# A fused convolution and two-layer block: TensorE's products of a step in another order, first-layer and second-layer products alternating

## The reference, cut to what matters

```python
# x (4, 4096, 192); weight_gen (4, 4096, 8 heads, 7 taps); w_in (192, 2048); w_out (2048, 192)
w = exp(weight_gen - max(weight_gen, -1)); w = w / (sum(w, -1) + 1e-9)
out[b, s, h, :] = sum over k of w[b, s, h, k] * x_pad[b, s + k, h, :]     # causal, 24 columns a head
x = out.reshape(16384, 192)
h = x @ w_in                                                             # first layer, 192 -> 2048
g = where(h >= 1, h, where(h <= -1, 0, (h + 1)**2 / 4))                  # gate
return g @ w_out                                                         # second layer, 2048 -> 192
```

## Time and profile before

| | |
|---|---|
| median of three runs | 1261.16 us |
| profiled execution, first to last instruction | 1259.3 us (its own time is not given apart from this span) |
| TensorE products | 1209.8 us, 96% of the span |
| TensorE weight loads | 1094.7 us, 87% |
| VectorE | 818.9 us, 65% |
| ScalarE | 898.3 us, 71% |
| GpSimd | 697.0 us, 55% |
| mean granted TensorE clock | 0.998 |

### The profile page before, as it was taken

How to read it: one execution, slowest core, us unless ns; L and a number is a source line. 1 busy time by engine, 2 the same in 40 slices (tenths; PEclk the granted TensorE clock), 3 DMA queues, 4 the chain that set the end, 5 groups by cost and what they waited for, 6 DMA issues and landing times.

```text
span 1259.3 us, 21159 instructions
## 1 busy us (share of the span) xinstructions
PE 1209.8 (96%) x6932; PEld 1094.7 (87%) x6932; DVE 818.9 (65%) x1434; ACT 898.3 (71%) x1773; POOL 697.0 (55%) x450
## 2 busy tenths in 40 slices
PE   0699999999999999999999999999999999999998
PEld 0578999999999999999999999999999999999987
DVE  1886666666666666666666666666666666666565
ACT  0567777777777777777777777777777777777776
POOL 2496555775555775555776555676555676555500
PEclk9999999999999999999999999999999999999999
DMA  3311111001111101111101111101111100110000
GB/s 116 105 36 48 49 48 48 27 20 47 47 47 47 44 3 47 47 47 47 47 0 47 47 47 47 47 8 39 47 47 47 47 20 27 47 47 12 13 13 13
DMA packets 17426, 51.59 MB, mean 41 GB/s; under 512 B 1800, under 2 KB 8068, under 8 KB 17408
## 3 DMA queue, kind: packets, MB, share of 16 engines
q1 hardware_dynamic: 17264, 51.25, 11.9%
q10 hardware_dynamic: 144, 0.11, 0.0%
HBM read 38.77 MB, written 12.58 MB: 41 GB/s over the span
## 4 chain that ended last, share of the span: by engine, by line
PE 93%; SPq 3%; DVE 3%; DMA 1%; ACT 1%; issue 0%; DVEq 0%
PE slot L581 46%; PE acc L601 44%; PE slot L566 2%; SPq L240 1%; SPq L255 1%; DMA out_raw<-in_moe_w_out 1%; SPq L252 1%; DVE slot L472 1%; DVE gate_low L478 1%; DVE out_parts L515 0%; DVE in_main_low L508 0%; SPq L258 0%; DVE in_rest_low L508 0%; ACT gate_high L375 0%; SPq L223 0%
## 5 line engine op out<-in xcount | busy, mean ns | idle before, releaser
L601 PE MATMUL acc<-out_parts,gate_high 128*128 128x384 f32 x2048 | 616.4, 357 | 6.0 <-DVE gate_low L478 5.9
L478 DVE TENSOR_TENSOR gate_low<-slot,gate_high 128x512 fp32r<-128x512 f32 x512 | 353.7, 691 | 398.9 <-ACT gate_high L375 398.6
L601 PE MATMUL acc<-out_parts,gate_low 128*128 128x192 f32 x2048 | 513.7, 251 | 0.5 <-DVE gate_low L478 0.5
L364 ACT ACTIVATE half_relu<-slot 128x512 f32<-128x512 f32 x512 | 307.7, 601 | 288.5 <-PE slot L581 288.4
L601 PEld LDWEIGHTS acc<-out_parts,gate_high 128*128 128x128 f32 x2048 | 384.9, 188 | 27.1 <-DVE gate_low L478 8.4
L601 PEld LDWEIGHTS acc<-out_parts,gate_low 128*128 128x128 f32 x2048 | 390.3, 191 | 17.9 <-DVE gate_low L478 0.7
L472 DVE SCALAR_TENSOR_TENSOR slot<-slot,square 128x512 f32<-128x512 f32 x512 | 353.0, 690 | 3.9 <-ACT square L370 3.9
L370 ACT ACTIVATE square<-half_relu 128x512 f32<-128x512 f32 x512 | 325.2, 635 | 0.0
L375 ACT ACTIVATE gate_high<-slot 128x512 fp32r<-128x512 f32 x512 | 304.0, 594 | 25.6 <-DVE slot L472 25.4
L301 POOL TENSOR_TENSOR conv<-x_in,tap_w 128x768 f32<-128x768 f32 x31 | 47.8, 1542 | 482.3 <-DVE tap_w L462 468.4
L301 POOL TENSOR_TENSOR tap<-x_in,tap_w 128x768 f32<-128x768 f32 x186 | 289.6, 1564 | 0.0
(11 more groups left out here) (41 smaller groups left out, 493.4 us busy)
## 6 DMA issues: line engine op xcount, KB each, us to landing
x_in<-in_x SPq DMA_DIRECT2D x30, 960.0 KB
out<-out_sb SPq DMA_DIRECT2D x32, 384.0 KB, 2.6
gen_in<-in_weight_gen SPq DMA_DIRECT2D x31, 112.0 KB, 2.3
out_raw<-in_moe_w_out SPq DMA_DIRECT2D x4, 384.0 KB, 9.9
in_main<-in_moe_w_in SPq DMA_DIRECT2D x4, 256.0 KB, 4.7
in_rest<-in_moe_w_in SPq DMA_DIRECT2D x8, 128.0 KB, 7.6
x_in<-in_x SPq DMA_DIRECT2D x1, 768.0 KB
x_in<-in_x SPq DMA_DIRECT2D x4, 139.5 KB
```

The costliest lines, as they stand in the source:

```text
L364: nc.scalar.activation(half_relu[n % 2][:], tile_slot(pair, b, n)[:], ACT.Relu, scale=0.5, bias=0.5).then_inc(relu_done, 1)
L478: nc.vector.tensor_tensor(gate_low[n % 4][:], tile_slot(pair, b, n)[:], gate_high[n % 4][:].bitcast(F32), ALU.subtract).then_inc(gate_low_ ...
L601: ins = nc.tensor.matmul(dst, stationary, moving, start=(n == 0 and j == 0), stop=(n == NT - 1 and j == 1))
```

## The change

The same products with the same operands are issued, as many as before. Only their order on TensorE is another:

- The five first-layer products of tile n and the eight second-layer products of tile n - 3 are now one mixed sequence, `hidden_and_outputs`. Neighbours write different banks, since the blocks of the second layer are staggered too.
- The transposes of `turn` stand behind the whole step. Before, they stood between the step's first and second layer.
- In the two places where only one layer is there (the first three steps of the kernel, the last three tiles) the products stand alone.

```diff
-            def hidden(pair, b, n):
-                slot_free(pe, pair, b, ("tile", n))
...
-                for j, (w, xt) in enumerate(products):
...
-                ins.then_inc(hidden_done, 1)
+            def hidden(pair, b, n, j):
+                if j == 0:
+                    slot_free(pe, pair, b, ("tile", n))
...
+                if j == 4:
+                    ins.then_inc(hidden_done, 1)
+
+            def out_ready(pair, b, n):
                 wait(pe, gate_low_done, pair, 2 * NT, NT * b + n + 1)
...
+            def acc_free(pair, b, n, i):
+                if n == 0:
+                    wait(pe, out_summed, pair, 2 * TOK, TOK * (b - 1) + i + 1)
+
+            def out_both(pair, b, n, i):
+                acc_free(pair, b, n, i)
+                ins = nc.tensor.matmul(acc[i][:, 0:2 * D], gate_high[n % 4][:, i * P:(i + 1) * P],
+                                       out_parts[:, n, :, :].rearrange("p a d -> p (a d)"),
+                                       start=(n == 0), stop=(n == NT - 1))
+                if n == NT - 1:
+                    ins.then_inc(acc_done, 1)
+
+            def out_low(pair, b, n, i):
+                nc.tensor.matmul(acc[i][:, 0:D], gate_low[n % 4][:, i * P:(i + 1) * P],
+                                 out_parts[:, n, 0, :], start=False, stop=False)
...
+            def hidden_and_outputs(pair, b, n, done):
+
+                if done[2] == NT - 1:
+                    hidden(pair, b, n, 0)
+                    out_ready(*done)
+                    out_low(*done, 0)
...
+                    hidden(pair, b, n, 4)
+                    out_low(*done, 2)
+                    out_low(*done, 3)
+                    out_both(*done, 2)
+                    out_both(*done, 3)
+                else:
+                    hidden(pair, b, n, 0)
+                    out_ready(*done)
+                    out_both(*done, 0)
+                    hidden(pair, b, n, 1)
+                    out_low(*done, 0)
+                    hidden(pair, b, n, 2)
+                    out_both(*done, 1)
+                    hidden(pair, b, n, 3)
+                    out_low(*done, 1)
+                    hidden(pair, b, n, 4)
+                    out_both(*done, 2)
+                    out_both(*done, 3)
+                    out_low(*done, 2)
+                    out_low(*done, 3)
...
                     for n in range(NT):
-                        hidden(pair, b, n)
+                        if n >= LAG:
+                            hidden_and_outputs(pair, b, n, (pair, b, n - LAG))
+                        elif not (b == 0 and is_first(pair)):
+                            hidden_and_outputs(pair, b, n, (*before(pair, b), NT + n - LAG))
+                        else:
+                            only_hidden(pair, b, n)
                         if n in turn_after(pair, b):
                             turn(*after(pair, b), turn_after(pair, b).index(n))
-                        if n >= LAG:
-                            outputs(pair, b, n - LAG)
-                        elif not (b == 0 and is_first(pair)):
-                            outputs(*before(pair, b), NT + n - LAG)
```

More of the change, by code:

```diff
@@ L568, in turn @@
                 ins.then_inc(turned, 1)
[L570 to L585 removed]
+            def hidden(pair, b, n, j):
+                if j == 0:
+                    slot_free(pe, pair, b, ("tile", n))
+                    if n == 0:
+                        wait(pe, turned_low_done, pair, 4, 2 * b + 2)
+                    if b == 0 and is_first(pair) and n % CT == 0:
+                        pe.wait_ge(in_low_done, 2 * (n // CT) + 2)
+                w, xt = ((in_main_high, xt_high), (in_main_low, xt_high), (in_main_high, xt_low),
+                         (in_rest_high, xt_rest), (in_rest_low, xt_rest))[j]
+                ins = nc.tensor.matmul(tile_slot(pair, b, n)[:], w[:, n * P:(n + 1) * P], xt[b][:],
+                                       start=(j == 0), stop=(j == 4))
+                if j == 4:
+                    ins.then_inc(hidden_done, 1)
+            def out_ready(pair, b, n):
                 wait(pe, gate_low_done, pair, 2 * NT, NT * b + n + 1)
@@ L590, in outputs @@
                     pe.wait_ge(out_low_done, n // CT + 1)
-                for i in range(TOK):
-                    tokens = slice(i * P, (i + 1) * P)
-                    if n == 0:
-                        wait(pe, out_summed, pair, 2 * TOK, TOK * (b - 1) + i + 1)
-                    low = (acc[i][:, 0:D], gate_low[n % 4][:, tokens], out_parts[:, n, 0, :])
-                    both = (acc[i][:, 0:2 * D], gate_high[n % 4][:, tokens],
-                            out_parts[:, n, :, :].rearrange("p a d -> p (a d)"))
-                    order = (both, low) if n < NT - 1 else (low, both)
-                    for j, (dst, stationary, moving) in enumerate(order):
-                        ins = nc.tensor.matmul(dst, stationary, moving, start=(n == 0 and j == 0),
-                                               stop=(n == NT - 1 and j == 1))
-                    if n == NT - 1:
-                        ins.then_inc(acc_done, 1)
+            def acc_free(pair, b, n, i):
+                if n == 0:
+                    wait(pe, out_summed, pair, 2 * TOK, TOK * (b - 1) + i + 1)
@@ new lines, in outputs @@
+            def outputs(pair, b, n):
+                out_ready(pair, b, n)
+                if n < NT - 1:
+                    out_both(pair, b, n, 0)
+                    out_both(pair, b, n, 1)
+                    out_low(pair, b, n, 0)
+                    out_both(pair, b, n, 2)
+                    out_low(pair, b, n, 1)
+                    out_both(pair, b, n, 3)
+                    out_low(pair, b, n, 2)
+                    out_low(pair, b, n, 3)
+                else:
+                    out_low(pair, b, n, 0)
+                    out_low(pair, b, n, 1)
+                    out_both(pair, b, n, 0)
+                    out_low(pair, b, n, 2)
+                    out_both(pair, b, n, 1)
+                    out_low(pair, b, n, 3)
+                    out_both(pair, b, n, 2)
+                    out_both(pair, b, n, 3)
@@ new lines, in only_hidden @@
+            def only_hidden(pair, b, n):
+                for j in range(5):
+                    hidden(pair, b, n, j)
+            def hidden_and_outputs(pair, b, n, done):
[17 more added lines that the diff above has]
+                    out_ready(*done)
+                    out_both(*done, 0)
+                    hidden(pair, b, n, 1)
+                    out_low(*done, 0)
+                    hidden(pair, b, n, 2)
+                    out_both(*done, 1)
+                    hidden(pair, b, n, 3)
+                    out_low(*done, 1)
+                    hidden(pair, b, n, 4)
[3 more added lines that the diff above has]
+                    out_low(*done, 3)
```

10 lines of the change are left out of this document (removed).

## The result

The changed kernel takes 1325.8 us (median of four runs, 1325.5 to 1327.1) against 1261.0 us before: a ratio of 1.0516, 95% interval 1.0501 to 1.0531. It is slower, as forecast, but 18 us more than the 1308 of the forecast and 2 us outside its range.

What follows compares the result with a forecast made beforehand. The prediction took TensorE, 93% of the span, as the bound, with no waits in the loop. From 1261.2 us it took -4 for pace, +49 for the stall and +2 for the start: 1308.2 us, range 1289 to 1324.

Steps and rivals of the forecast that it cites:

- The stall at a group's start: Steps 2 and 3 of groups 1 to 31: TensorE waits for VectorE's sums, 1.58 us each, +49 us.
- The pace: Ordinary mixed steps: 8 ns gained in each of 509 steps, -4 us, bounds -18 and +8.
- the change of bank is no cheaper than staying: First steps of the kernel: products changing bank cost 0.23 us like the others, so alternation gains near nothing.
- The lower bound: Best case for the pace in ordinary steps: 0.036 us a step gained, -18 us.
- The start: Group 0, waits for `gate_low`: four products now stand behind the wait, +2 us, bounds +0.9 and +4.
- Ordinary tiles: Loop tiles away from group starts: 1.08 us to spare remains, no wait, priced at nothing.
- The clock: TensorE's clock through the new 1.5 us stalls: stays at 1.00 from 110 us on, no cost.
- The first (products become cheaper): Rival, all steps: alternating banks saves 0.15 us a step, -76 us instead of -4, giving 1236 us; chance 0.08.
- The stalls did not lower the clock: Rival, group starts: stalls halve the clock for 3.2 us, 31 times, +50 us, giving 1358 us; chance 0.05.
- the wait does not recur in every step: Rival, ordinary steps: another 0.3 us wait in half of a group's steps, +77 us, giving 1385 us; chance 0.03.
- the stall is there: Rival, group starts: no stall because the sums come earlier than derived, 1257 to 1262 us; chance 0.02.

Runs made afterwards that it cites:

- B0 alone: Kernel before, with only step 3 of every group in the mixed order and the transposes behind it: 1294.7 us.
- H5 alone: Changed kernel with step 3 of every group back in the order of before, the last first-layer product of step 2 staying late: 1285.5 us.
- the transposes alone: Kernel before, with only the transposes moved behind the second layer: 1263.7 us, ratio 1.0019.
- with steps 2 and 3 as before: Changed kernel with steps 2 and 3 of every group in the order of before, layers apart: 1275.0 us.
- the kernel with two blocks: Kernel before, layers apart, with each step's four 384-column products issued first and then its four 192-column products: 1265.2 us.
- batching two tiles: Kernel before, changed to issue two tiles at a time, with eight gate buffers and the sums one step later: 1258.0 us, ratio 0.9972.
- the widened kernels: 192-column products widened to 384 columns: 1400.4 us in the order of before, 1409.2 us in the mixed order (steps 2 and 3 of a group unmixed).
- the mixed kernel with equal lengths: Changed kernel with products 512 columns long (group 0 and tile 15 keep 384) and steps 2 and 3 of a group unmixed: 1580.1 us.

## Why the prediction was wrong

- **The stall at a group's start: right.** +49 forecast; 31 x 1.57 = 48.7 measured by step 3, 50 by the pair of steps. Place, releaser and the number of waits came out, each link of the chain within 0.03 us and TensorE's arrival within 0.05. Kernels that moved one part at a time confirmed it: B0 alone +33 us, H5 alone 0.27 us a group, the transposes alone +2.4, and with steps 2 and 3 as before no wait.
- **The pace: the step that failed.** I put it at -4 us with bounds of -18 and +8. It is +0.46 a group, 31 x 0.46 = +14 (13 by the other split): outside the bounds and of the other sign. The argument was "the change of bank is no cheaper than staying", and that holds. But I took the bank for the only thing that an order can change. The rows for it were from a stretch in which all products are 512 columns long, the one case without the effect. And I bounded the loss by the spread of distances inside the old order, which cannot show what a new order does. The excess of 231 over 227, which I let stand unexplained, was the effect itself: with all products at 512 columns and the order of before it is gone. (The lower bound also has a slip. Five H at 5 ns and four B at 4 make 0.041 us a step, not 0.036, so -21 us; it does not bear on the miss, which lies at the other end.)
- **The start: +2 forecast, about +0.8 measured** at the start of group 1, and another 0.7 at the end that I had not counted. That the two together come near +2 is luck.
- **Ordinary tiles: right.** From 130 to 1240 us TensorE's only wait is the one for `out_sb`; none for `gate_low` or for a slot appears.
- **The clock: right.** The granted clock stays at its higher level through the stalls, 1.00 in each of these windows of the changed kernel. The first holds the wait of 454.81, the others nearly all of them. (The one low stretch stands in the start, as before: 0.50 from 54.0 to 55.5 us and 0.64 from there to 58.0, behind a wait of 4.6 us.)

```profile
450.00:460.00 10.00, 8.64 (x51) 7.54 (x51) 6.32 (x13) 6.84 (x16) 2.37 (x2) 1.00 0.35 108
110.00:600.00 490.00, 473.70 (x2682) 424.28 (x2682) 307.48 (x546) 344.72 (x681) 277.79 (x176) 1.00 0.11 37
600.00:1300.00 700.00, 675.36 (x3821) 604.51 (x3820) 435.40 (x769) 491.97 (x973) 364.96 (x231) 1.00 0.10 34
```

- **The rivals.** The first (products become cheaper) had the sign of the pace wrong, as I had. A cost of writing one bank twice does not show here (2.287 us a step with five changes of bank or with nine). The stalls did not lower the clock, the wait does not recur in every step, and the stall is there: the other three fell as well. The Trainium skill, TensorE: Matmul & The Clock Gate, section Back-to-back issue gap, gives 216 ns for isolated products of 512 columns; with a weight load before each, no steady stretch of these runs is below 226.

**What stays open.** Shown is that the excess follows the sequence of lengths and nothing else that was tried. Why TensorE needs longer behind a change of length is not shown. No law for its size is shown either: the number of changes of length does not order the steps (3 in the kernel with two blocks, 2.294 us; 9 before, 2.287), the extra on short products in a row (108 to 112) overlays it, and the same order settles in either of two patterns (2.307, or 2.311 and 2.336 in turn), by a choice that I cannot predict.

## What to carry to other kernels

When products move, ask first who waits for the last product of each chain and what stood before the first product that waits: here one product later in one step and one earlier in the next cost 50 us through a chain on two other engines that nobody touched. In this kernel, products of one length issued in long runs were cheaper than the same products in alternation: batching two tiles gained 0.3%, interleaving the layers cost about 1% by the pace alone. A mean over steps can hide two patterns, so look at the single steps before comparing means. A price for an order should not be read from a stretch that lacks what the order changes.

## What was not expected of the hardware

- TensorE's stream with a weight load before each product ran at 226 to 227 ns for 512 columns and 173 for 384 only well inside a run of equal lengths. Behind a change of length products take up to 12 ns more in the widened kernels (185 instead of 173, 238 instead of 227), and H3 up to 16 more (243) in the changed order with step 3 apart. How long this lasts differs: three products in the kernel with two tiles at a time, four in the second layer of the widened kernel, ten behind the transposes of the mixed kernel with equal lengths.
- This pace did not depend on how much ScalarE and VectorE worked (74% and 66% busy, or 30% and 31%), nor on which PSUM bank neighbours write. With the layers apart the distances were equal to the nanosecond; in the mixed order the same step lengths came back within 1 or 2 ns.
- One order of products can run in either of two stable patterns, 2.307 or 2.324 us a step on average, each held from one set of transposes to the next.
